# Three matmul stages regrouped into four stages of seven Strassen products each, with weight items and hidden activations kept in DRAM

## What is computed

```python
kv = np.einsum('bhsd,bhse->bhde', k, v)
out = np.einsum('bhsd,bhde->bhse', q, kv)
rms = np.sqrt(np.mean(out * out, axis=-1, keepdims=True) + 1e-06)
x = out / rms * g_norm                        # then reshaped to (4608, 512)
gate = 1.0 / (1.0 + np.exp(-(x @ w_gate)))    # w_gate, w_val: 512 x 1536
x = gate * (x @ w_val) @ w_mid                # 1536 x 512 (moe_w_out)
h = x @ w_in                                  # 512 x 2048
g = np.where(h > 0.0, h, np.exp(np.minimum(h, 0.0)) - 1.0)
return g @ w_out                              # 2048 x 512
```

## Time and profile before

| what | value |
|---|---|
| median of 3 runs | 1837.48 us (1836.17 to 1838.25) |
| the profiled execution, its own time | 1837.31 us |
| its span, first to last instruction | 1835.5 us |
| PE busy | 1807.7 us, 98% |
| DVE / ACT / POOL busy | 741.7 / 387.8 / 81.9 us |
| TensorE clock granted, mean | 0.997 of full speed |
| DMA | 93.74 MB, mean 51 GB/s |

### The profile page before, as it was taken

One profiled execution on the slowest core, in us unless ns is written; L12 is line 12 of the kernel. 1 busy time (PEld: TensorE's weight loads), 2 busy tenths in 40 slices (PEclk: granted clock), 3 DMA queues, 4 the chain that ended last, 5 costly groups with the idle time before them and its releaser, 6 DMA issues.

```text
span 1835.5 us, 21760 instructions
## 1 busy us (share of the span) xinstructions
PE 1807.7 (98%) x8304; PEld 1504.7 (82%) x8304; DVE 741.7 (40%) x1240; ACT 387.8 (21%) x710; POOL 81.9 (4%) x117
## 2 busy tenths in 40 slices
PE   7998999999999999999999999999999999999999
PEld 6887888888888888888888888888888888888887
DVE  3676532222222222212222376454545454444443
ACT  6784310101111010101010232121212121211111
POOL 3552000000000000000000000000000000000000
PEclk9999999999999999999999999999999999999999
DMA  9895420000101010101010132010101010101000
GB/s 235 246 277 184 131 75 1 32 14 2 44 0 46 0 46 0 46 0 46 0 46 0 59 124 69 1 46 0 46 0 46 0 46 0 46 0 46 1 22 23
DMA packets 69792, 93.74 MB, mean 51 GB/s; under 512 B 4736, under 2 KB 43648, under 8 KB 69760
## 3 DMA queue, kind: packets, MB, share of 16 engines
q1 hardware_dynamic: 69232, 92.29, 16.6%
q10 hardware_dynamic: 528, 1.05, 0.2%
HBM read 65.01 MB, written 28.31 MB: 51 GB/s over the span
## 4 chain that ended last, share of the span: by engine, by line
PE 90%; DMA 1%; DVE 1%; issue 0%; ACT 0%; POOL 0%; SPq 0%; POOLq 0%; ACTq 0%; DVEq 0%
PE bank L470 53%; PE bank L487 37%; DMA qkv<-in_k_dram 0%; DMA w_raw<-in_moe_w_in_dram 0%; DVE o L681 0%; ACT y L627 0%; POOL sq L393 0%; PE bank L420 0%; DMA x_gated<-y 0%; DMA out_dram<-y 0%; PE bank L438 0%; PE bank L429 0%; DVE w_pre L701 0%; DVE x_hl L695 0%; PE bank L439 0%
## 5 line engine op out<-in xcount | busy, mean ns | idle before, releaser
L470 PE MATMUL bank<-x_hl,w_rest 128*128 128x512 f32 x3024 | 713.2, 389 | 0.0
L470 PEld LDWEIGHTS bank<-x_hl,w_rest 128*128 128x128 f32 x3024 | 567.8, 188 | 117.7
L487 PE MATMUL bank<-w_rest,u_hl 128*128 128x512 f32 x1620 | 386.3, 389 | 0.8 <-DVE u_hl L712 0.8
L487 PEld LDWEIGHTS bank<-w_rest,u_hl 128*128 128x128 f32 x1620 | 304.0, 188 | 64.2 <-issue 1.2
L719 DVE TENSOR_TENSOR u_f<-bank,act_f 128x512 f32<-128x512 f32 x108 | 74.7, 691 | 618.9 <-PE bank L470 618.9
L470 PE MATMUL bank<-x_hl,w_pre 128*128 128x512 f32 x1296 | 302.3, 389 | 2.0 <-DVE x_hl L695 1.3
L470 PEld LDWEIGHTS bank<-x_hl,w_pre 128*128 128x128 f32 x1296 | 243.0, 188 | 53.4 <-DVE x_hl L695 2.2
L487 PE MATMUL bank<-u_hl,w_rest 128*128 128x512 f32 x1188 | 282.4, 389 | 0.0
L487 PEld LDWEIGHTS bank<-u_hl,w_rest 128*128 128x128 f32 x1188 | 223.0, 188 | 46.2
L613 ACT ACTIVATE act_f<-act_f 128x512 f32<-128x512 f32 x144 | 91.0, 632 | 591.8 <-DVE act_f L733 591.8
L733 DVE TENSOR_SCALAR act_f<-bank 128x512 f32<-128x512 f32 x144 | 99.4, 690 | 270.4 <-PE bank L470 270.4
(11 more groups left out here) (50 smaller groups left out, 666.2 us busy)
## 6 DMA issues: line engine op xcount, KB each, us to landing
qkv<-in_q_dram SPq DMA_DIRECT2D x32, 288.0 KB, 5.2
qkv<-in_k_dram SPq DMA_DIRECT2D x32, 288.0 KB, 5.7
qkv<-in_v_dram SPq DMA_DIRECT2D x32, 288.0 KB, 6.1
x_attention<-o SPq DMA_DIRECT2D x32, 288.0 KB, 3.6
x_gated<-y SPq DMA_DIRECT2D x36, 256.0 KB, 2.0
x_raw<-x_gated SPq DMA_DIRECT2D x9, 1024.0 KB, 5.2
out_dram<-y SPq DMA_DIRECT2D x36, 256.0 KB, 2.0
x_raw<-x_attention SPq DMA_DIRECT2D x8, 1024.0 KB, 5.2
```

What stands on the lines that cost most here:

```text
L470: mm = pe.matmul(dst[:, :], w[:, a, m * P:(m + 1) * P], x_hl[:, m, b, :], start=(m == 0 and a == b == 0), stop=(m == KT - 1 and a == 1))
L487: mm = pe.matmul(ACC[m][:, :], lhs, rhs, start=(j == 0 and a == b == 0), stop=(j == tiles - 1 and a == 1))
```

## The change

Everything from the end of attention on is new. There are now four stages, one after the other, each for all tokens: gate and val (stage 1), mid (stage 2), in (stage 3), out (stage 4). Between them the activations go through DRAM: `u_gated` (1536 x 4608) and `u_elu` (2048 x 4608) beside `x_gated`. A unit is a 2 x 2 block product C = A B, with tokens and features halved, done as seven products P1 to P7 instead of eight. A are the activations (A11, A12, A21, A22: x and hidden units, halved in tokens and in the summed features), B are the weights.

* Stage 1 has 36 units, stage 2 has 6, stage 3 has 24, stage 4 has 18. A product of stages 1 and 3 is 12 matmuls of 384 columns (`hidden_product`, L912), of stage 2 it is 36 (`mid_product`, L945), of stage 4 it is 24 matmuls of 256 columns (`out_product`, L977).
* The order is P1, P2, P6, P5, P7, P3, P4, each into one of PSUM's pairs of banks `PA` (two, in turn), `PB`, `PC`. P6, P7 and P4 are added on top of what `PA` holds, P3 on `PB`. Before each such addition ACT copies the state out (a snapshot, `s_snap`), and DVE adds `PC`, `PA` or `PB` to the copies (`combine`, L1380) for C11, C22 and C12. C21 is what `PA` holds at the end.
* The sums of activations (S1 to S4) are made by DVE in stages 1 and 3 and by GpSimd in stages 2 and 4 (`mid_sums`, `out_sums`). The sums of weights are made by GpSimd for all 19 chunks (`weight_sums`). Each item is then split into high and low as before, into a ring of SBUF slots for activations.
* The weights are split during stage 1, between the other steps of a unit (`fill1`). The items of chunks 3 and later are stored to `weight_items` in DRAM (`store_weight`) and loaded again when their stage comes. Two buffers `out_w` hold items on their way: the third item of a chunk waits for the first one's store.

In the diff, cut to its core, `vis = n // 3` and `j = n % 3` in stage 1; the first part is SP's, `mid_sums` GpSimd's (`out_sums` is the same with 8 x 128 elements), `wait_target` and `hidden_product` TensorE's, and the rest ScalarE's. A slot for an item of stage 2 is free when the item two before has been used.

```diff
+    P1, P2, P6, P5, P7, P3, P4 = range(ITEMS)
+    NT = 384
+    CHUNK_UNIT = {1: 0, 2: 1, 3: 3, 4: 4, 5: 6, 6: 7, 7: 9, 8: 10, 9: 12, 10: 13, 11: 15,
+                  12: 21, 13: 22, 14: 24, 15: 25, 16: 27}
...
+                if j == 0 and vis + 1 < VISITS1:
+                    sp.wait_ge(s_lo, split1(vis, P4))
+                    load_x(x1_dram, (vis + 1) % NS)
+                for c, at in ((2, 0), (3, 1), (4, 3), (5, 4), (6, 6), (7, 7), (8, 9), (9, 10), (10, 12), (11, 13),
+                              (12, 18), (13, 19), (14, 22), (15, 24), (16, 25)):
+                    if n == at:
...
+                        load_chunk(c)
...
+                for i in (0, 1):
+                    store_weight(n, i)
+                store_gated(n, "11")
+                for i in (2, 3, 4):
+                    store_weight(n, i)
+                store_gated(n, "22")
+                store_weight(n, 5)
+                store_gated(n, "12")
+                store_weight(n, 6)
+                store_gated(n, "21")
...
+            def mid_sums(vis):
...
+                pool.wait_ge(s_k0, 16 * (vis + 1))
+                pool.tensor_tensor(A21_2, A11_2, A21_2, ALU.subtract).then_inc(s_usum, 1)
+                pool.wait_ge(s_a22, 16 * (vis + 1))
...
+                pool.tensor_tensor(sum_2[:, :, :], raw_22[:, :, :], A21_2, ALU.subtract).then_inc(s_usum, 1)
...
+                pool.wait_ge(s_lo, split2(vis, P1, 2))
+                pool.tensor_tensor(A11_2, sum_2[:, :, :], A11_2, ALU.add).then_inc(s_usum, 1)
+                pool.wait_ge(s_lo, split2(vis, P2, 2))
+                pool.tensor_tensor(raw_12[:, :, :], raw_12[:, :, :], sum_2[:, :, :], ALU.subtract).then_inc(s_usum, 1)
...
+            def wait_target(n, i):
...
+                if i == P1 and n >= 2:
+                    pe.wait_ge(*c21_taken(n - 2))
+                if i == P2 and n >= 1:
+                    pe.wait_ge(s_comb, comb(n - 1, "11"))
+                if i == P6:
+                    pe.wait_ge(s_snap, snap(n, P1))
+                if i == P5 and n >= 1:
+                    pe.wait_ge(s_comb, comb(n - 1, "12"))
+                if i == P7:
+                    pe.wait_ge(s_snap, snap(n, P6))
+                if i == P3:
+                    pe.wait_ge(s_snap, snap(n, P5))
+                if i == P4:
+                    pe.wait_ge(s_comb, comb(n, "22"))
...
+            def hidden_product(n, i, cell, slot):
...
+                for g in range(2):
+                    for kt in range(2):
...
+                        for a, b in PARTS:
+                            mm = pe.matmul(dst[:, g, 0:NT], w[:, a, cols], ring[:, slot, b, kt, :],
...
+            def split_weight(c, i):
...
+                if c >= DIRECT and stored(c, i) >= 2:
+                    act.wait_ge(s_wst[stored(c, i) % 2], 16 * (stored(c, i) // 2))
...
+            def split_u1(vis, i, t):
...
+                if ITEMS * vis + i >= 2:
+                    act.wait_ge(s_prod, prod(FIRST2, ITEMS * vis + i - 2))
...
+            def gated_unit(n):
...
+                fill1(n, 0)
+                act.wait_ge(s_prod, prod(n, P1))
+                wait_count(act, s_u, comb(n - 1, "11"))
+                act.activation(s1[:, :, :], pa[:, :, 0:NT], ACT.Copy).then_inc(s_snap, 1)
+                fill1(n, 1)
+                act.wait_ge(s_comb, comb(n, "11"))
+                act.activation(s1[:, 0, :], s1[:, 0, :], ACT.Sigmoid).then_inc(s_sig, 1)
+                fill1(n, 2)
+                act.wait_ge(s_prod, prod(n, P6))
+                wait_count(act, s_u, comb(n - 1, "12"))
+                act.activation(s2[:, :, :], pa[:, :, 0:NT], ACT.Copy).then_inc(s_snap, 1)
+                fill1(n, 3)
...
```

1281 lines of the change are left out of this document (937 added, 344 removed).

## The result

The changed kernel takes 1855.08 us (median of 4 runs, 1854.67 to 1858.80), the kernel before 1837.57 us on the same chip. The ratio is 1.0101 with a 95% interval of 1.0083 to 1.0118. The prediction was 1774 us, 1700 to 1835: wrong in the time and in the sign.

What follows compares the result with a forecast made beforehand. The prediction took PE's matmuls to bound the kernel: 1837.3 - 166.3 (matmuls) + 57.8 (SP's queue) + 7 (clock) + 24.6 (GpSimd's sums in stage 2) + 6 (turn) + 8 (starts) = 1774.4 us, range 1700 to 1835.

Steps and rivals of the forecast that it cites:

- The matmuls: All four stages: seven products for eight, 173.3 ns per 384-column and 120.0 ns per 256-column matmul, removing 166.3 us.
- the fixed surcharge: TensorE: each matmul carries 13.3 ns besides one column a cycle at 2.4 GHz, whatever its columns.
- The rival of the smaller surcharge: TensorE: N/2.4 + 2.5 ns a matmul, 162.5 and 109.2 ns, gain 24 us larger, 1750 us; chance 0.03.
- SP's queue and its clock: Stage 1: weight stores wait behind loads, delaying P6's copy and P7, 57.8 us; half clock after such gaps, 7 us.
- The clock: Stage 1: half clock after eight long gaps of PE, 0 to 3 us each, 7 us in all.
- The mid stage: Stage 2: GpSimd's sums and DVE's low parts exclude each other, PE idles 4.1 us a visit, 24.6 us for 6.
- The turn: From attention to stage 1: uncovered chain 1.2, late copy by ACT 3.0, DVE's added work 2; 6 us, bounds 3 and 15.
- the 172.6 us: Profiled time before outside back-to-back matmuls: attention, turn to the first layer, tail and what lies around the span.
- The starts: Stages 3 and 4 and three stage starts from DRAM: late ACT and load latency, together 8 us, bounds 3 and 20.
- The code mostly issues early: Starts of three stages from DRAM: each costs a load latency mostly issued early; part of the 8 us term.
- Slower than before: Stages 2 and 4: GpSimd's sums reach the time before at 3.4 ns an element, 1916 us at 4; chance 0.12.
- heavier: Sums at 6.3 us, 1 KB pieces at 300 GB/s, turn 15 us, 3 us clock per gap: 1830 us; chance 0.08.

## Why the prediction was wrong

**The matmuls** (-166.3 us) were right: 173 and 120 ns, so the fixed surcharge read off 288 and 512 columns holds at 256 and 384. The rival of the smaller surcharge, 162.5 and 109.2 ns, is out.

**The mechanisms** of stages 1 and 2 and of the turn were named as they then appeared, and the experiments bear them out. What failed is the size of four terms, the queue's, the clock's, the mid stage's and that of the starts, all to the same side.

**SP's queue and its clock** (57.8 + 7): in stage 1 the units behind the turn lost 98 us, 67.6 of them in PE's 14 waits for the copy of P6 and most of the rest at half clock behind these. Units 3, 6, 9, 12 and 24 waited 6.4 to 6.9 us, where 7.0 were forecast, and those with x alone 3.8 to 4.6, for 4.2. The chunk-only units were priced at 1.7 us and waited 3.2 to 4.4. The sum counted from an empty queue, while the last weight and result stores of the unit before were still in it. The trace fits that: in unit 4 the last of these landed 3.0 us after the first raw load was issued, and the first weight store landed 6.7 us after its issue, against 2.8 in the median of all.

**The clock** (7 us) was the worst term, a factor of six: 40 us in all stages. The step that failed is the count. I counted eight gaps in stage 1, none in the mid stage, though my own sum for the queue had 14. There were 14 waits for the copy of P6 alone, and one to three more in every visit of the mid stage. The trace shows 26 us of half-clock steps in stage 1, 9 in the mid stage, 5 in stages 3 and 4. The price of a gap was put at 0 to 3 us; beyond the wait itself each of the 14 cost 1.4 to 2.5.

**The mid stage** (24.6): 41.1 us. Sums of 5.16 to 5.79 us were as taken. But the working laid only three sums and nine low parts end to end and asked when the ninth is due. PE met the block earlier: in visits 1 to 5 it waited 1.1 to 1.4 us for the fourth low part (the first third of P2), then 3.3 to 3.4 for the fifth, then ran at half clock. A sum that fits on average still stops whoever needs the next item. (That GpSimd's longest such instruction of before is 0.8 us was misread as well: its low parts of the squares take up to 0.99.)

**The turn** (6, bounds 3 and 15) held within its bounds. Unit 0 lost 20.8 us, but 9.0 us were lost at the same place before, inside the 172.6 us that the sum carries along, so the change added 11.8. PE's wait for the copy of P1 was forecast (3.0 us; it was 4.2), but the 8 us of added DVE work were put mostly into its idle time. They stand ahead of the scalings in DVE's order, so PE waited for these, 2.57 us the first time, with the clock at 0.51 for 14 us, the wait for the copy among them.

**The starts** (8, bounds 3 and 20): 35 us. Stage 3 lost 19.6 (its start 5.5, ACT's exponentials ahead of the next copy 0.8 in two units of four, the last three units 4.5), stage 4 lost 15.1 at its first unit. "The code mostly issues early" is the step that failed: SP came to the second raw load of the out stage only 11.1 us into the stage, since 3.6 MB of cells for each of the last three units and the stores behind them stood in front of it, and it landed 14.1 us later.

Queue and clock of stage 1 (33), mid stage with its clock (17), turn (6) and starts (27) are 83 us short, which is the 81 us between 1774 and 1855 to within 2.

**The rivals.** "Slower than before" had 0.12, all of it on GpSimd's rate, from 3.4 ns an element; it measured 2.24 to 2.5 in the mid stage and 2.5 to 3.0 in the out stage, and cost nothing more. The nearest was "heavier", 1830 us: every cost at its upper end. It had 0.08, and slower by its way had none.
